# Two feed-forward layers behind an attention: each layer in two phases through DRAM, its second product by Strassen's seven products

## The reference, cut to what matters

```python
def _moe_ref(x, w_in, w_out):                      # layer 0, x: 2304 x 512
    h = x @ w_in                                   # 512 -> 2048
    g = np.where(h >= 1, h, np.where(h <= -1, 0.0, (h + 1) ** 2 / 4))
    return (g @ w_out).astype(np.float32)          # 2048 -> 512

def _moe2_ref(x, w_in, w_out):                     # layer 1, same sizes
    h = x @ w_in
    g = np.maximum(h, 0.0) + np.log1p(np.exp(-np.abs(h)))
    return (g @ w_out).astype(np.float32)

def reference(**kwargs):
    attn_out = _attn_ref(q, k, v)                  # 4 batches, 8 heads, 576 rows, 64 wide, k and v pooled by 8
    x = attn_out.transpose(0, 2, 1, 3).reshape(2304, 512)
    return _moe2_ref(_moe_ref(x, ...), ...)
```

## Time and profile before

| | |
|---|---|
| median of 3 runs | 914.42 us (913.91 to 915.57) |
| profiled execution: span | 909.9 us |
| PE busy | 882.0 us (97%) |
| PEld / DVE / ACT / POOL busy | 828.2 / 447.5 / 416.1 / 371.9 us |
| DMA | 36.06 MB, mean 40 GB/s |

### The profile page before, as it was taken

The page is one execution under the profiler, slowest core; times in us unless marked ns, Lnnn a source line. Parts: engine busy times, 40 slices in busy tenths (PEclk is TensorE's granted clock), DMA queues, the critical chain, the costliest instruction groups (busy, mean ns, idle before and its releaser), DMA issues.

```text
span 909.9 us, 14298 instructions
## 1 busy us (share of the span) xinstructions
PE 882.0 (97%) x4914; PEld 828.2 (91%) x4914; DVE 447.5 (49%) x778; ACT 416.1 (46%) x857; POOL 371.9 (41%) x313
## 2 busy tenths in 40 slices
PE   7887899999999999999999999999999999999997
PEld 7665799999999999999999999999989999998996
DVE  4999755322322322322355754545545554544543
ACT  3788654232232232322354654544554554544443
POOL 6999553242242232242343343343343343443332
PEclk9999999999999999999999999999999999999999
DMA  8973243000000000000043100100100100100101
GB/s 178 215 185 117 70 130 125 24 1 1 1 0 0 0 0 0 0 0 0 24 137 118 47 1 1 35 0 0 35 0 0 35 0 0 35 0 0 36 1 35
DMA packets 54975, 36.06 MB, mean 40 GB/s; under 512 B 20640, under 2 KB 46240, under 8 KB 54944
## 3 DMA queue, kind: packets, MB, share of 16 engines
q1 hardware_dynamic: 54944, 35.66, 14.3%
HBM read 30.93 MB, written 4.72 MB: 39 GB/s over the span
## 4 chain that ended last, share of the span: by engine, by line
PE 91%; DVE 4%; ACT 2%; issue 1%; DMA 1%; SPq 0%; POOL 0%; DVEq 0%; ACTq 0%
PE ps L720 44%; PE ps L741 22%; PE ps L743 22%; PE ps L666 2%; ACT qT L351 1%; PE ps L693 1%; DVE v_sum L499 1%; DMA q_raw<-in_q_dram 1%; PE ps L652 1%; DVE k_sum L499 1%; DVE den L543 1%; DVE prob L562 0%; DVE pmax L519 0%; ACT kT L355 0%; DVE prob L527 0%
## 5 line engine op out<-in xcount | busy, mean ns | idle before, releaser
L304 POOL TENSOR_TENSOR g_lo<-act_a,g_hi 128x384 fp32r<-128x384 f32 x192 | 240.9, 1255 | 462.7 <-ACT g_hi L411 462.7
L720 PE MATMUL ps<-x_hi,w_split 128*128 (+1 forms) x1536 | 391.4, 335 | 0.3 <-DVE prob L527 0.3
L720 PEld LDWEIGHTS ps<-x_hi,w_split 128*128 128x128 f32 x1536 | 279.6, 188 | 9.9 <-issue 0.9
L720 PE MATMUL ps<-x_lo,w_split 128*128 (+1 forms) x768 | 257.8, 336 | 0.0
L741 PE MATMUL ps<-g_hi,w_split 128*128 128x384 f32 x768 | 194.7, 334 | 0.0
L743 PE MATMUL ps<-w_split,g_hi 128*128 128x512 f32 x576 | 179.3, 392 | 0.9 <-POOL g_lo L304 0.9
L720 PEld LDWEIGHTS ps<-x_lo,w_split 128*128 128x128 f32 x768 | 144.1, 188 | 0.0
L580 DVE TENSOR_SCALAR act_a<-ps 128x384 f32<-128x384 f32 x96 | 53.5, 558 | 179.0 <-PE ps L720 179.0
L431 ACT ACTIVATE act_a<-act_a 128x384 f32<-128x384 f32 x96 | 50.5, 526 | 193.5 <-DVE act_a L580 193.5
L741 PEld LDWEIGHTS ps<-g_hi,w_split 128*128 128x128 f32 x768 | 138.6, 188 | 0.0
L741 PE MATMUL ps<-g_lo,w_split 128*128 128x384 f32 x384 | 128.3, 334 | 0.0
(11 more groups left out here) (49 smaller groups left out, 700.5 us busy)
## 6 DMA issues: line engine op xcount, KB each, us to landing
w_raw<-in_moe_w_in_dram SPq DMA_DIRECT2D x32, 256.0 KB, 2.7
w_raw<-in_moe_w_out_dram SPq DMA_DIRECT2D x32, 256.0 KB, 3.0
k_raw<-in_k_dram SPq DMA_DIRECT2D x16, 288.0 KB
q_raw<-in_q_dram SPq DMA_DIRECT2D x32, 144.0 KB, 5.6
v_raw<-in_v_dram SPq DMA_DIRECT2D x16, 288.0 KB
out_dram<-X SPq DMA_DIRECT2D x18, 256.0 KB, 2.7
```

Of the source, the lines that this page charges most:

```text
L304: nc.gpsimd.tensor_tensor(g_lo[:, slot, :], act_a[:, slot, :], g_hi[:, slot, :].bitcast(F32), ALU.subtract).then_inc(g_lo_done, 1)
L720: last = mm(ps[:, H_BANK[f % HB], 0:TT], w_split[:, f, part, w], buf(x, t, c), start=c == 0 and a == 0, stop=c == KC - 1 and a == 2)
```

## The change

Each layer now runs in two phases over three tiles of 768 tokens.

**Phase 1** makes all of h and g. A step is a pair: one block of 128 features by 768 tokens, as two matmuls of 384 columns in each of 12 places (`make_h`, L1007 of the new file), 48 pairs a layer. The element-wise operations are 768 wide. Two pairs (feature blocks j and j + 8) make a quad; its four 384-wide blocks are G11, G12 (token halves by feature halves), G21, G22. POOL makes four sums of them (`s_sums`): S1 = G21 + G22, S3 = G11 - G21, S2 = S1 - G11, S4 = G12 - S2. Seven of the eight blocks go to DRAM in one store (`gops`), by SP, one store a quad, 24 a layer. `ops` has three slots.

**Phase 2** is the second product as Strassen's (Winograd's form) seven block products. For each product p and each of the three tiles SP loads an operand of 128 x 3072 from `gops`; ACT splits hi and DVE lo in four pieces of 768 into one of two buffers `xs`; 48 matmuls of 384 columns multiply it by a sum of quarters of w_out (`product`, L1025). Those sums T are made by POOL (`t_sums`), split by ACT and DVE (`hi_t`, `lo_t`). DVE adds the result into the blocks of X (`add_y`). In layer 1 the finished blocks are transposed on TensorE (`turn_y`, 12 times 6 transposes), copied by ACT and stored.

The memory of w_split now holds W (the first product's weights only) and, over parts of it, T and the raw quarters of w_out. The next layer's weights are loaded at the end of phase 2.

The core of the diff:

```diff
+            def store_ops(layer, k):
+
+                u, i, j = use_of(layer, k), k // JJ, W_ORDER[layer][k % JJ]
+                sp.wait_ge(s_added, 4 * (layer * QUADS + k + 1))
+                sp.dma_start(gops[layer][:, i, :, j, :].rearrange("a p t -> p a t"), ops[:, u % SLOTS, 0:PRODUCTS, :]
+                             ).then_inc(ops_stored[u % SLOTS], 16)
+
+            def load_ops(layer, m):
+
+                u, (p, i) = use_of(layer, QUADS + m), divmod(m, NT)
+                sp.wait_ge(*slot_free(u))
...
+                sp.dma_start(ops[:, u % SLOTS, :, :], gops[layer][p, i, :, :, :]).then_inc(ops_loaded[u % SLOTS], 16)
...
+            for layer in range(2):
+                for k in range(QUADS):
...
+                    store_ops(layer, k)
+                for r in range(3):
+                    load_raw(layer, r)
+                for m in range(STEPS):
+                    load_ops(layer, m)
...
+            def s_sums(layer, k):
+
+                n, slot = layer * QUADS + k, use_of(layer, k) % SLOTS
+                pool.wait_ge(g_made, 2 * n + 2)
+                nc.gpsimd.tensor_tensor(ops[:, slot, S1, :], ops[:, slot, G21, :], ops[:, slot, G22, :], ALU.add
+                                        ).then_inc(s_added, 1)
+                nc.gpsimd.tensor_tensor(ops[:, slot, S3, :], ops[:, slot, G11, :], ops[:, slot, G21, :], ALU.subtract
+                                        ).then_inc(s_added, 1)
+                pool.wait_ge(s_added, 4 * n + 1)
...
+                pool.wait_ge(s_added, 4 * n + 3)
...
+                    s_sums(layer, k)
+                    if 2 <= k % JJ < 2 + PIECES and k // JJ + 1 < NT:
+                        fill_lo_piece(fill_of(layer, k // JJ + 1), k % JJ - 2)
...
+            def exp_abs(a):
+
+                n, t = HPAIRS + a, t_a[:, a % 2, :, :]
+                act.wait_ge(h_done, n + 1)
+                act.wait_ge(g_made, n - 1)
+                nc.scalar.activation(t, bank_pair(v_of_pair[n]), ACT.Abs).then_inc(h_abs, 1)
...
+                nc.scalar.activation(t, t, ACT.Exp, scale=-1.0).then_inc(u_made, 1)
...
+            def softplus(a):
+
+                n = HPAIRS + a
+                u, b = t_a[:, a % 2, :, :], t_b[:, a % 2, :, :]
+                dve.wait_ge(u_made, a + 1)
+                dve.wait_ge(g_made, n - 1)
+                nc.vector.tensor_scalar(b, u, 1.0, None, ALU.add).then_inc(b_made, 1)
+                dve.wait_ge(b_made, a + 1)
+                nc.vector.scalar_tensor_tensor(out=u, in0=b, scalar=1.0, in1=u, op0=ALU.subtract, op1=ALU.subtract
+                                               ).then_inc(r_made, 1)
+                if a > 0:
+                    total(a - 1)
+                dve.wait_ge(r_made, a + 1)
+                nc.vector.scalar_tensor_tensor(out=u, in0=bank_pair(v_of_pair[n]), scalar=0.0, in1=u,
+                                               op0=ALU.max, op1=ALU.subtract).then_inc(s_made, 1)
...
+                else:
+                    for k in range(6):
+                        hi_w(1, k)
+                    for piece in range(PIECES):
+                        fill_hi_piece(fill_of(1, 0), piece)
+                    hi_w(1, 6)
+                    hi_w(1, 7)
...
+                for j in range(JJ):
...
+                    for d in range(2):
+                        for s, (part, g_part) in enumerate(((0, 0), (1, 0), (0, 1))):
+                            last = mm(banks[:, d, :], Tm[:, t, part, j, d * P:(d + 1) * P],
+                                      g[:, g_part, j * TB:(j + 1) * TB],
+                                      start=j == 0 and s == 0, stop=j == JJ - 1 and s == 2)
```

## The result

| | before | after |
|---|---|---|
| median | 915.0 us (913.91 to 916.21, 4 runs) | 1012.45 us (1011.01 to 1015.93, 4 runs) |
| span of the profiled execution | 909.9 us | 1011.4 us |

The ratio is 1.107, interval 1.103 to 1.111: slower by 97 us. The forecast was 1017 us, range 950 to 1062.

The account below looks back on a forecast made before the run. The prediction took TensorE to bound the kernel, busy 882.0 of 909.9 us. Its terms, from -50.3 us for removed matmuls to +100.4 for layer 1's first phase, summed to +102.6 on 914.4: 1017 us, range 950 to 1062.

Parts of the forecast that it names:

- The bound and the pace: Whole kernel: TensorE is the bound and pays 0.452 ns a column; fewer second-product matmuls give -50.3 us.
- Seam of layer 0: Between layer 0's phases: TensorE waits for last sums, stores, w_out loads and the first operand; +31.0 us.
- Layer 1's first phase: Layer 1's phase 1 with its seam: a 4.30 us pair loop plus POOL's sums outlast TensorE's work; +100.4 us.
- a 768-wide x_lo piece stands behind S4 and adds that: 12.2 us: Layer 1's phase 1: in 8 of 24 quads this POOL piece adds 1.8 us to a 10.4 us quad.
- POOL's sums run in one block: Layer 1's phase 1: POOL's queue leaves no gap, DVE's SBUF work waits; a quad costs 10.4 us.
- Phase 2: Second products: DVE, ACT and loads fit within TensorE's 8.33 us step, once each product barely; +1 us.
- Layer 0 to layer 1: Change of layers: eight weight quads through two buffers delay TensorE; +6.3 us, ends 0 and 12.
- Attention's end: End of attention: POOL's x_lo pieces double, but lo_w(1) and lo_w(2) leave POOL; -1 us.
- Clock: TensorE after the two long pauses: lower clock for some us, 3 us lost in each; +6 us.
- A: Rival, layer 1's phase 1: POOL's sums slip between DVE's operations, a pair costs 4.35 us; 962 us, chance 0.17.
- B: Rival, both seams: DVE and ACT keep TensorE's pace, operand load passes w_out loads; about 914 us, chance 0.04.
- C: Rival: large transfers at 237 GB/s, POOL's sums stretched by DVE, clock low longer; +54, 1071 us, chance 0.11.

Follow-up runs that it names:

- e4: New kernel with SP issuing the three w_out quarter loads one each ahead of the last three stores of phase 1, not behind the last; 990.39 us.
- e9: New kernel with SP's order around the seam raw 0, store 21, load 0, raw 1, store 22, load 1, store 23, load 2, raw 2; 991.66 us.
- e1: New kernel with POOL's four sums of layer 1 cut to 8 columns from 384, so the result is not the reference; 975.71 us.
- e10: New kernel, layer 1's phase 1: b made by ACT instead of DVE, Ln of the pair before ahead of Exp, DVE's total first; 974.53 us.
- e2: New kernel with one line moved: DVE runs the total of the pair before ahead of b and r instead of behind them; 1005.44 us.
- e3: New kernel with SP issuing each result store of layer 1 one step later, waiting for step m-4's copy instead of m-3's; 993.66 us.
- e12: New kernel with layer 1's x filled before weight quads 2 to 7 are split, and quads 4 to 7 loaded and split between first pairs; 1032.23 us.
- e7: New kernel with POOL's order at attention's end changed: x_lo pieces and the first w_lo stand singly between the sums of v; 1012.66 us.

## Why the prediction was right, and where it was right by luck

**The bound and the pace.** Right. TensorE pays for columns: 1008 matmuls in 174.97 us when nothing interrupts (predicted 174.9). The 4.19 us given there for the old softplus are 4.17 by the same pace (12 x 0.1735 + 9 x 0.232); nothing rests on the difference.

**Seam of layer 0.** 31.0 predicted, 29.5 measured, and by the steps named: SP's rows of the new kernel have the stores to 316.49, the three quarters to 322.68, and only then the first operand's load. The last store goes 6.9 us after TensorE's last matmul (7.0 predicted), the first fill starts at 335.06, 19.0 us later (22.1 predicted), and TensorE 3.5 us after that (1.9 predicted): the bytes were quicker, the fill slower. The bytes moved at 328 to 430 GB/s against the 300 taken. The Trainium skill (HBM Reference, Specifications (TRN2)) gives about 425 GB/s for a core that streams alone; the window from 330 us, at 430, agrees, so that sentence was the better one for that stretch. Over the whole way from the last store to the first fill neither was: that rate would give 16.1 us, the sum had 22.1, and 19.0 were measured. e4 proves that w_out's place in the queue is a part, e9 that the last stores and their slots come next.

**Layer 1's first phase.** Right in mechanism, proved by e1 (33 us are POOL's sums, the loop alone is 4.24 us a pair against 4.30 worked out) and e10. Wrong in one step: "a 768-wide x_lo piece stands behind S4 and adds that: 12.2 us". It added nothing: a quad is 10.10 us with or without it. The piece runs from 568.96 to 571.52 and is only in the way of SBUF work of DVE, and in that time DVE ends the total, has s (from PSUM) and then waits for Abs and Exp. The 24 quads come to 242 us, not 264: 14 us of that are this step, 7 the 0.3 us by which 10.10 is under 10.4. e2 shows the other side: once that gap is closed, the piece does cost 1.5 us a quad.

The 10.10 itself has luck in it. The forecast let POOL's sums run in one block, with b behind the third and r behind the fourth. In the quad above b, r and the total stood between the sums, and both sides were stretched: counted from S1's start b ended at 2.4 us (3.4 predicted), r at 4.1 (5.1), the total at 5.8 (6.1). That the sums hold the loop up is right, how they do it was not.

**Phase 2.** "It fits, once each product barely: +1 us" is the step that failed: 15 us. I counted each engine's time in a step, and did not walk SP's queue, where a store of results waits for ACT up to 26 us ahead of operand loads. e3 shows it by taking it away: no wait is left in that phase.

**Layer 0 to layer 1.** 6.3 predicted, 9.1 measured, between its ends of 0 and 12. That the chain of weight quads is what holds it is shown by the pause going in e12. I did not take the 2.8 us apart.

**Attention's end.** -1 predicted, +3.4 measured, with other executions of the same code 8 us apart. The place was read off the profile (the last v_sum), but where the doubled x_lo pieces would land was not: two of them and the first w_lo stand in a row, with a sum of v before them, where a v_sum is due. e7 did not give it back, so where the 4 us belong stays open.

**Clock.** 3 us a pause predicted; 2.5 in layer 0's seam, 1.5 in layer 1's. The term was short because the two unforeseen waits in phase 2 each brought their own, 1.7 and 2.8 us: 48 matmuls took 11.35 us after one, 8.57 in the others.

**The rivals.** A (sums slip in between, 962) is refuted by r's 1.66 and the total's 1.76 us. B (faster) needed seams under 19 us with the loads passing the queue, and a loop at or below 4.16; the loop is 4.24 and the seam 29.5. e9's order makes the first pause that short, yet the pause came back in two more pieces. C had worse sharing on the wrong side: transfers were faster than the forecast, not slower; POOL's sums were stretched (S2 1.33 and S4 1.60 us), but inside a quad shorter than forecast.

## What to carry to other kernels

Fewer matmuls only pay if what fed them still fits beside what is left: here 50 us of TensorE were removed, and with them the time under which layer 1's softplus, the stores and the loads had hidden. Walk each queue in written order, the DMA queue first, and ask of each wait what stands behind it; the three cheapest gains here (store one step later, quarters ahead of the last stores, b on another engine) were all changes of place. And check a sum's terms one by one even when the total fits.

## What the runs showed that I had not expected

- DVE and POOL took turns in layer 1. r (566.46, 1.66 us) ends 0.8 us after S2, S4 (1.60 in place of 1.01) after r by a similar amount, and so on: one instruction each, both stretched. I had modelled POOL's queue as leaving no gap. In attention, v_sum did wait for several POOL instructions on end (6.65 us, where others took 0.28). What tells the two cases apart was not tested.
- A pause of 7 us can cost as much clock as one of 29: 2.8 us after 7.08 (48 matmuls in 11.35 against 8.57) and 1.7 after 7.88, 2.5 after 29.45; e9's row at 957.22 had 9.98 for 48 after 7.25, so 1.4.
- A DRAM round trip through three slots of 1.4 to 1.6 MB took 11 to 14 us a slot while both directions were busy (e9), though stores had a median of 5.1 us to landing and loads one of 7.0 in the same run.
